# Rows of x: written in token order and gathered per expert tile, instead of scattered into expert order

## The chip, the core and the metric

The kernel runs on one core of a Trainium2 chip. The metric is the device time of one execution in microseconds (us). PE is TensorE, DVE is VectorE, ACT is ScalarE, POOL is GpSimd, SP is the sync engine, which here only starts DMA transfers.

## What is computed

Attention without a softmax, then a mixture of 8 experts in which each token goes to one expert, then a gated linear layer:

```python
kv = np.einsum('bhsd,bhse->bhde', k, v)                 # batch 8, heads 8, seq 576, dim 64
out = np.einsum('bhsd,bhde->bhse', q, kv)
x = out / sqrt(mean(out * out, axis=-1) + 1e-6) * g_norm  # as [4608, 512]
logits = x @ w_gate + modality_bias[modality_id]         # 8 experts
e_idx = argmax(logits); gate = softmax(logits)[e_idx]
for e in range(8):                                       # 512 -> 1024 -> 512
    out[e_idx == e] = gate * (relu(x[e_idx == e] @ w1[e]) @ w2[e])
out = (sigmoid(out @ wg_gate) * (out @ wg_val)) @ w_out  # 512 -> 1536 -> 512
```

Products with large weights are made in three passes of float32r parts (high times high, high times low, low times high), so "high" and "low" copies are made of weights and activations.

## The kernel before, in words

There are three stages on the same engines, each engine with its own instruction stream.

**Attention.** 36 steps ("slots" run from 0 to 42, with fixed lags) treat 72 chunks of 128 half tokens, two chunks a slot: partitions 0 to 63 hold the first four heads of 64 tokens and partitions 64 to 127 the other four heads of the same tokens. In a slot PE makes the output of one pair of chunks (L1006), transposes the q of a later one (L1029), ACT squares the output, copies the transposed q (L566) and prepares the next q (L584), DVE sums the squares (L828), takes the reciprocal (L808), writes the normalised rows to `xb` (L815) and the scaled products with the gate weights to `lgh` (L822). At the start of a batch of 4.5 slots PE makes k times v with 144 small matmuls (L1042). SP loads k, v and q of a batch and raw expert weights, all on its one queue.

**Routing.** The 72 chunks form nine groups of 4, 8, 12, 12, 12, 8, 8, 4, 4 (`GROUPS`). When a group's last chunk is done, PE folds the two halves into logits (L1060, 5 slots later), DVE finds the expert and counts (`route_part`, slot 6), PE ranks over the partitions (L1066, L1067), and DVE computes each token's row in its expert's region of the DRAM tensor `x_rows` (`place_part`, slot 7, last instruction L793). POOL then issues one indirect DMA per chunk (L462), 128 rows of 1088 bytes each: half of x, and behind it the token's number. `xb` holds 36 chunks, so a group's rows wait there for their places. After the last group, the token counts are turned into tables (L837 to L860), and eight DMAs of zeros fill each expert's last, partly filled tile (`zero_pads`, L385, four from SP and four from ACT), each behind a register load. Then the first tile of x can be read.

**Experts.** 40 tiles of 128 rows. POOL reads a tile with four plain DMAs (`load_x`, L482), reads its token numbers (`load_tok`, L486), gathers their gates with an indirect DMA (`gather_gate`, L490) and scatters the finished rows (`scatter`, L496). DVE turns x (`x_turned`), makes low parts, splits the next expert's weights (L740, L746), and multiplies with the gate (`y_of`). PE multiplies (L1090 up, L1112 down). The loop over the full tiles is a hardware loop with two tiles in its body; the first tile and the last ones are written out.

**Gated layer.** Nine blocks of 512 tokens (L1136 and L1147), at the end of which POOL scatters each 128 rows by `out_tok`.

Waits are on semaphores. SP's and POOL's streams are in program order: what stands behind a wait waits too.

## Time and profile before

| what | value |
|---|---|
| median of 3 runs | 1635.85 us (1634.67 to 1637.78) |
| profiled execution, its time | 1633.38 us |
| profiled execution, its span | 1631.4 us |
| mean granted clock of PE | 0.948 |
| busy share of the span: PE, DVE, ACT, POOL | 92%, 36%, 23%, 19% |

The span is from the first to the last instruction; the 2.0 us between it and the execution's time lie around it. A busy share is a mean over three stages that are limited in different ways, so the stages have to be read one by one. In the rows, "idle before <-issue" is time in which an engine waited for nothing that the profile shows.

### The profile page before, as it was taken

How to read it: one execution, taken by the hardware profiler on the slowest of the kernel's cores; microseconds unless marked ns; L12 is line 12 of the kernel's file. 1: busy time of each engine (PE TensorE's matmuls, PEld its weight loads, DVE VectorE, ACT ScalarE, POOL GpSimd, SP SyncE). 2: the span in 40 equal slices, each digit the busy share in tenths (PEclk: the TensorE clock that was granted, in tenths of full speed). 3: DMA queues.
4: the chain of work that ended last, by engine and by line, in shares of the span. 5: the costliest groups of instructions: out<-in, count | busy, mean ns of one | idle time of the engine just before them, and what ended most of it. 6: DMA issues, size and time to landing. Idle time of an engine off the chain costs nothing.

```text
span 1631.4 us, 25528 instructions
## 1 busy us (share of the span) xinstructions
PE 1505.4 (92%) x8836; PEld 1234.1 (76%) x8837; DVE 584.1 (36%) x1095; ACT 380.4 (23%) x698; POOL 311.8 (19%) x402
## 2 busy tenths in 40 slices
PE   5765549999999999989999999999999999999997
PEld 4544438888888888868888888888888888888885
DVE  4444366457645665334411212122121211212111
ACT  4443312222221212223311211112121111212111
POOL 0223354444444444310000000000000000000000
PEclk8676559999999999999999999999999999999998
DMA  9555234245423443315300201002010100100000
GB/s 330 202 210 187 72 124 146 75 116 150 127 84 97 138 122 96 102 57 127 80 27 1 52 1 27 27 2 51 0 27 27 27 26 0 27 26 1 26 0 26
DMA packets 78612, 124.07 MB, mean 76 GB/s; under 512 B 17342, under 2 KB 41918, under 8 KB 78528
## 3 DMA queue, kind: packets, MB, share of 16 engines
q1 hardware_dynamic: 56576, 80.85, 16.8%
q0 software_dynamic: 17216, 39.75, 7.6%
q10 hardware_dynamic: 4736, 2.26, 0.6%
q8 instruction: 63, 1.03, 0.3%
q14 instruction: 21, 0.17, 0.0%
HBM read 91.38 MB, written 32.52 MB: 76 GB/s over the span
## 4 chain that ended last, share of the span: by engine, by line
PE 88%; issue 6%; DVE 2%; ACT 1%; DMA 1%; another core or an unknown queue 1%; SPq 0%; POOLq 0%; POOL 0%; ACTq 0%; DVEq 0%
PE ps L1136 37%; PE ps L1147 18%; PE ps L1112 13%; PE ps L1090 13%; PE ps L1042 2%; PE ps L1099 2%; PE ps L1029 1%; PE ps L1006 1%; DMA vt<-in_v 1%; ACT qp L584 0%; DVE ew L746 0%; DMA x_rows<-zero 0%; DVE xb L815 0%; DVE ssum L828 0%
## 5 line engine op out<-in xcount | busy, mean ns | idle before, releaser
L1136 PE MATMUL ps<-yhi,gv 128*128 128x512 f32 x1728 | 557.0, 393 | 6.5 <-DVE wo L967 5.8
L1136 PEld LDWEIGHTS ps<-yhi,gv 128*128 128x128 f32 x1728 | 325.3, 188 | 79.2 <-DVE wo L967 6.2
L1136 PE MATMUL ps<-ylo,gv 128*128 128x512 f32 x864 | 339.4, 393 | 0.0
L1147 PE MATMUL ps<-wo,shi 128*128 128x512 f32 x864 | 266.8, 390 | 1.4 <-DVE slo L984 1.4
L982 DVE TENSOR_TENSOR s<-ps,sig 128x512 f32<-128x512 f32 x108 | 74.7, 691 | 472.0 <-ACT sig L666 467.3
L1090 PE MATMUL ps<-ew,xhi 128*128 x640 | 202.4, 397 | 4.5 <-DVE xlo L891 3.2
L529 POOL DMA_INDIRECT out<-ot,out_tok x36 | 34.5, 960 | 870.4 <-ACT ot L681 864.6
L1112 PE MATMUL ps<-ew,hhi 128*128 x640 | 197.1, 389 | 1.3 <-DVE hlo L908 1.3
L1136 PEld LDWEIGHTS ps<-ylo,gv 128*128 128x128 f32 x864 | 162.6, 188 | 37.8 <-issue 1.1
L1147 PEld LDWEIGHTS ps<-wo,shi 128*128 128x128 f32 x864 | 162.1, 188 | 36.9 <-DVE slo L984 1.9
L666 ACT ACTIVATE sig<-ps 128x512 f32<-128x512 f32 x108 | 64.5, 597 | 494.8 <-PE ps L1136 486.1
L1147 PE MATMUL ps<-wo,slo 128*128 128x512 f32 x432 | 168.3, 390 | 0.0
L984 DVE TENSOR_TENSOR slo<-s,shi 128x512 fp32r<-128x512 f32 x108 | 74.8, 692 | 214.5 <-ACT shi L669 214.5
L1112 PEld LDWEIGHTS ps<-ew,hhi 128*128 128x128 f32 x640 | 120.1, 188 | 26.4 <-issue 1.5
L1090 PEld LDWEIGHTS ps<-ew,xhi 128*128 128x128 f32 x640 | 118.0, 189 | 29.0 <-issue 6.1
L1090 PE MATMUL ps<-ew,xlo 128*128 x320 | 125.7, 393 | 0.0
L1112 PE MATMUL ps<-ew,hlo 128*128 x320 | 124.8, 390 | 0.0
L669 ACT CAST shi<-s 128x512 fp32r<-128x512 f32 x108 | 67.1, 622 | 226.7 <-PE ps L1147 225.9
L482 POOL DMA_DIRECT2D xg<-x_rows x160 | 90.8, 568 | 150.0 <-issue 145.1
L462 POOL DMA_INDIRECT x_rows<-xb,r_idx x72 | 69.5, 965 | 156.9 <-DVE r_idx L793 137.1
L1147 PEld LDWEIGHTS ps<-wo,slo 128*128 128x128 f32 x432 | 81.1, 188 | 17.1
L746 DVE SCALAR_TENSOR_TENSOR ew<-raw,g_tab,ew 128x1024 f32 (+1 forms) x64 | 82.2, 1284 | 8.4 <-DVE ew L740 4.3
(159 smaller groups left out, 1214.8 us busy)
## 6 DMA issues: line engine op xcount, KB each, us to landing
raw<-in_moe_w SPq DMA_DIRECT2D x64, 512.0 KB
xg<-x_rows POOLq DMA_DIRECT2D x160, 64.0 KB
kt<-in_k SPq DMA_DIRECT2D x8, 1152.0 KB, 5.7
vt<-in_v SPq DMA_DIRECT2D x8, 1152.0 KB, 9.6
qt<-in_q SPq DMA_DIRECT2D x8, 1152.0 KB, 5.4
yin<-y_rows SPq DMA_DIRECT2D x32, 256.0 KB, 5.3
graw<-in_moe_w_gate SPq DMA_DIRECT2D x6, 512.0 KB, 3.8
graw<-in_moe_w_val SPq DMA_DIRECT2D x6, 512.0 KB, 4.8
```

What stands on the lines that cost most here:

```text
L462: nc.gpsimd.indirect_dma_start(out=x_rows, out_offset=bass.IndirectOffsetOnAxis(ap=r_idx[:, c:c + 1], axis=0), in_=xb[:, c % RING, :], in_ ...
L482: nc.gpsimd.dma_start(xg[32 * g:32 * g + 32, t.p], src.rearrange("(t j) x -> j t x", j=32)).then_inc(x_in[t.p], 16)
L529: nc.gpsimd.indirect_dma_start(out=out, out_offset=bass.IndirectOffsetOnAxis(ap=out_tok[:, 4 * b + m:4 * b + m + 1], axis=0), in_=ot[:, m] ...
L666: nc.scalar.activation(sig[:], ps[:, 2 * (f % 2), :], ACT.Sigmoid).then_inc(sig_made, 1)
L669: nc.scalar.copy(shi[:], s32[:]).then_inc(shi_made, 1)
L746: made = nc.vector.scalar_tensor_tensor(out=lo_part, in0=raw[:, u, cols], scalar=g_tab[:, bass.ds(qn % 4, 1)], in1=hi_part.bitcast(F32), o ...
L982: nc.vector.tensor_tensor(s32[:], ps[:, 2 * (f % 2) + 1, :], sig[:], ALU.mult).then_inc(s_made, 1)
L984: nc.vector.tensor_tensor(slo[:], s32[:], shi[:].bitcast(F32), ALU.subtract).then_inc(slo_made, 1)
L1090: last = mm(ps[:, 1 + f, :], x[:, t.p, rows], weights(e, c, part, cols), start=first, stop=end)
L1112: last = mm(ps[:, 5, :], x[:, rows], weights(e, DC + c // 2, part, cols), start=first, stop=end)
L1136: last = mm(ps[:, 2 * (f % 2) + part, :], gv[f // 2][:, w, part, d, cols], x[c % 2][:, d, :], start=first, stop=end)
L1147: last = mm(ps[:, 4 + m, :], s[:, rows], wo[f // 2][:, w, f % 2], start=(f == 0 and s is shi and w == 0), stop=(f == GC - 1 and s is slo))
```

## The change

The rows of x no longer go to expert order in DRAM. SP stores each pair of chunks as it is finished, in token order and without the token number (36 stores, 40 DMAs, of 256 KB a pair; a row of x is split into four rows of 512 bytes); `xb` shrinks to 8 chunks. `xb` is written after `lgh` instead of before it, and PE's next output waits for `xb`. There are six groups of 12 chunks.

To know which token stands where in expert order, a token list is built: for each pair of chunks POOL makes three one-hot tiles (`hots`: 128, 288 and 288 columns, bf16) from the place's remainder and quotient by 128, with the token's number split in two parts as factor; PE adds their products up over the group (12 matmuls, 9 slots after the group's end), DVE adds the group to `order` (10 slots). For the last group POOL and DVE make three pairs each. Then four matmuls with selection matrices and four DVE instructions turn `order` into row addresses (`row_of`), and each tile's column is copied to `row_now` (`aim`) and `seat_now` (`seat_aim`) by DVE with a column number from a register.

In the expert stage POOL issues four indirect gathers of 512-byte rows for a tile of x; the read of token numbers is gone. The zero pads are gone. `compact_rows` is moved behind the first two `x_turned`. At the eighth step of the first gated block DVE turns list numbers into token numbers (`tokens`, five instructions). SP's loads of attention are written out slot by slot among the stores.

```diff
-    CAP = N + 128
-    XW = D // 2 + 16
+    CAP = (N + 127) // 128 * 128
...
+    HALF = D // 2
...
-    RING = 36
+    RING = 8
...
-    GROUPS = [(0, 4), (4, 8), (12, 12), (24, 12), (36, 12), (48, 8), (56, 8), (64, 4), (68, 4)]
+    GROUPS = [(c, 12) for c in range(0, T, 12)]
...
-    LAG_RANK, LAG_PLACE = LAG_LG + 1, LAG_LG + 2
-    SLOTS = S + LAG_PLACE
+    LAG_RANK, LAG_PLACE, LAG_ORDER, LAG_KEEP = LAG_LG + 1, LAG_LG + 2, LAG_LG + 4, LAG_LG + 5
+    SLOTS = S + LAG_KEEP
+    LAST = len(GROUPS) - 1
...
+    x_v = x_rows.rearrange("(b p j g) x -> b p j (g x)", b=BATCH, j=J, g=2)
...
-    x_row = keep("x_row", [1, NT + 1], I32)
-    pad_row = keep("pad_row", [1, E], I32)
-    zero = keep("zero", [128, 2 * XW], F32)
+    x_col = keep("x_col", [1, NT + 1], I32)
+    seat_of = keep("seat_of", [128, QN], U32)
+    row_of = keep("row_of", [128, 4, QN], U32)
...
-    xb = att("xb", [128, RING, XW], F32)
+    xb = att("xb", [128, RING, HALF], F32)
...
-        def zero_pads(engine, e):
-            row = engine.value_load(pad_row[0:1, e:e + 1], min_val=e * CAP, max_val=e * CAP + N)
-            engine.dma_start(x_v[bass.ds(row, 128)].rearrange("w n x -> w (n x)"), zero[:]).then_inc(pads_out[0 if e == 0 else 1], 16)
+        def hots(engine, g, k):
+            pair = PG * g + k
+            engine.tensor_scalar(hot_r[:, k, :], across[:, 0:128], spot_r[:, g % 2, k:k + 1], None, ALU.is_equal)
+            engine.tensor_scalar(hot_q[:, k, 0, :], across[:], spot_q[:, g % 2, k:k + 1], seat_low[:, pair:pair + 1], ALU.is_equal, ALU.mult)
+            return engine.tensor_scalar(hot_q[:, k, 1, :], across[:], spot_q[:, g % 2, k:k + 1], seat_high[:, pair:pair + 1], ALU.is_equal, ALU.mult)
         @block.sync
...
+            def load_kv(b):
...
                 load(vt, v_v, b, v_in)
-                if b >= 2:
-                    sp.wait_ge(qp_made, (J * (b - 1) + 1) // 2)
-                load(qt, q_v, b, q_in)
-                if 1 <= b <= EARLY:
-                    load_raw(sp, 0, b - 1)
+            def store(o):
+                sp.wait_ge(x_normed, 2 * o + 2)
+                at = 2 * o % RING
+                b, j = 2 * o // J, 2 * o % J
+                if spans_two(o):
+                    sp.dma_start(x_v[b, :, j], xb[:, at, :]).then_inc(x_out[o % (RING // 2)], 16)
+                    sp.dma_start(x_v[b + 1, :, 0], xb[:, at + 1, :]).then_inc(x_out[o % (RING // 2)], 16)
+                else:
+                    sp.dma_start(x_v[b, :, j:j + 2], xb[:, at:at + 2, :]).then_inc(x_out[o % (RING // 2)], 16)
+            load_kv(0)
+            load(qt, q_v, 0, q_in)
+            load_kv(1)
+            load(qt, q_v, 1, q_in)
+            load_raw(sp, 0, 0)
+            load_kv(2)
+            for s in range(S + LAG_NORM + 1):
...
+                    if s == (J * (b - 1) + 1) // 2:
+                        sp.wait_ge(qp_made, s)
+                        load(qt, q_v, b, q_in)
+                        if b <= EARLY:
+                            load_raw(sp, 0, b - 1)
+                        if b + 1 < BATCH:
+                            load_kv(b + 1)
+                o = s - LAG_NORM - 1
+                if o >= 0:
+                    store(o)
             for unit in range(EARLY, UNITS):
                 load_raw(sp, 0, unit)
-            sp.wait_ge(pads_made, 1)
...
-            for e in range(E // 2):
-                zero_pads(sp, e)
             sp.wait_ge(gates_made, 1)
-            sp.dma_start(gates.rearrange("(b p j) a -> p b (j a)", p=R, j=J), r_val[0:R].rearrange("p (b j) -> p b j", b=BATCH)).then_inc(gates_out, 16)
+            sp.dma_start(gates_v, r_val[:].rearrange("p (b j) -> p b j", b=BATCH)).then_inc(gates_out, 16)
             sp.wait_ge(gates_out, 16)
...
+                pool.wait_ge(iota_made, 9 + n)
+                nc.gpsimd.iota(seat_i[R * n:R * n + R], [[2 * SEQ, BATCH], [1, J]], base=0, channel_multiplier=J).then_inc(iota_made, 1)
+            pool.wait_ge(iota_made, 11)
+            pool.wait_ge(seat_made, 1)
+            for g in range(len(GROUPS)):
+                wait(pool, pe_order, g)
+                pool.wait_ge(spot_made, g + 1)
+                for k in range(PG // 2 if g == LAST else PG):
+                    hots(nc.gpsimd, g, k).then_inc(hot_made, 1)
+            for n in range(RING // 2):
+                pool.wait_ge(x_out[n], stored(S - RING // 2 + n))
             def when(sem_, count):
                 wait(pool, sem_, count)
                 pool.sem_inc(turn, 1)
-            def row_of(t):
-                return pool.value_load(x_row[0:1, bass.ds(t.n, 1)], min_val=0, max_val=E * CAP - 128)
-            def load_x(t, row=None):
+            def load_x(t):
                 when(xt_made, t.n - 1)
-                row = row_of(t) if row is None else row
-                for g in range(4):
-                    src = x_v[bass.ds(row, 128), g // 2, 128 * (g % 2):128 * (g % 2) + 128]
-                    nc.gpsimd.dma_start(xg[32 * g:32 * g + 32, t.p], src.rearrange("(t j) x -> j t x", j=32)).then_inc(x_in[t.p], 16)
-            def load_tok(t):
-                row = row_of(t)
-                nc.gpsimd.dma_start(tok_now[:, t.p:t.p + 1], tok_v[bass.ds(row, 128)], allow_slow_non_contiguous=True).then_inc(t_in[t.p], 16)
+                when(aim_made, t.n + 1)
...
+                        in_offset=bass.IndirectOffsetOnAxis(ap=row_now[:, t.p, m:m + 1], axis=0)).then_inc(x_in[t.p], 16)
             def gather_gate(t):
-                when(t_in[t.p], 16 * (t.half + 1))
+                when(seat_aimed, t.n + 1)
                 nc.gpsimd.indirect_dma_start(
                     out=gate_now[:, t.p:t.p + 1], out_offset=None, in_=gates,
-                    in_offset=bass.IndirectOffsetOnAxis(ap=tok_now[:, t.p:t.p + 1], axis=0)).then_inc(gate_in[t.p], 16)
+                    in_offset=bass.IndirectOffsetOnAxis(ap=seat_now[:, t.p:t.p + 1], axis=0)).then_inc(gate_in[t.p], 16)
...
-            load_x(Tile(0, 0), 0)
+            load_x(Tile(0, 0))
             pool.sem_inc(x_asked, 1)
             pool.wait_ge(tables_made, 1)
-            pool.wait_ge(pads_out[1], 16 * (E - 1))
...
                     use(Tile(i, c - 2), scatter)
-                use(Tile(i, c), load_tok)
-                if c > 0:
-                    use(Tile(i, c - 1), gather_gate)
+                use(Tile(i, c), gather_gate)
             for n in range(2):
...
-            pool.wait_ge(tok_in, 16)
+            pool.wait_ge(tok_step, 5)
...
-            act.wait_ge(pads_made, 1)
-            for e in range(E // 2, E):
-                zero_pads(act, e)
...
+                wait(dve, pe_order, g - 1)
+                for n in range(2):
+                    part = slice(R * n, R * n + R)
+                    then(nc.vector.tensor_copy(spot_i[part], r_p[part, 0:m].rearrange("p (k two) -> p k two", two=2)[:, :, n]))
+                then(nc.vector.tensor_scalar(spot_qi[:], spot_i[:], 7, None, ALU.logical_shift_right))
+                nc.vector.tensor_copy(spot_q[:, g % 2], spot_qi[:])
+                nc.vector.scalar_tensor_tensor(out=spot_r[:, g % 2], in0=spot_qi[:], scalar=-128.0, in1=spot_i[:],
+                                               op0=ALU.mult, op1=ALU.add).then_inc(spot_made, 1)
+                if g == LAST:
+                    dve.wait_ge(spot_made, g + 1)
+                    wait(dve, pe_order, g)
+                    for k in range(PG // 2, PG):
+                        hots(nc.vector, g, k).then_inc(last_hot_made, 1)
             steps[0] = 0
             def then(ins):
                 chain(route_step, ins)
+            def keep_order(g):
+                dve.wait_ge(pe_order, g + 1)
+                if g == 0:
+                    kept = nc.vector.tensor_copy(order[:], ps[:, 3, ORDER])
+                else:
+                    dve.wait_ge(order_kept, g)
+                    kept = nc.vector.tensor_tensor(order[:], order[:], ps[:, 3, ORDER], ALU.add)
+                kept.then_inc(order_kept, 1)
...
+                if s - LAG_KEEP in ENDS:
...
-                        old = group_of(2 * o - RING)
-                        dve.wait_ge(x_out[old], 16 * GROUPS[old][1])
                     dve.wait_ge(rstd_made, o + 1)
...
-                            outs(o)[:, :, jj, 0:DH].rearrange("p h (g i) -> p h g i", g=2),
-                            scale[:, :, jj].unsqueeze(2).unsqueeze(3).to_broadcast([128, PAIRS, 2, 32]), ALU.mult).then_inc(x_normed, 1)
                     g = group_of(2 * o)
                     wait(dve, pe_lg, g - 1)
                     at = 2 * o - GROUPS[g][0]
                     nc.vector.tensor_tensor(lgh[:, g % 2, :, at:at + 2, :], outs(o)[:, :, :, DH:KX],
                                             scale.unsqueeze(3).to_broadcast([128, PAIRS, 2, E]), ALU.mult).then_inc(lgh_made, 1)
+                    if o >= RING // 2:
+                        dve.wait_ge(x_out[o % (RING // 2)], stored(o - RING // 2))
+                    for jj in range(2):
+                        nc.vector.tensor_tensor(
+                            xb[:, 2 * o % RING + jj, :].rearrange("p (g h i) -> p h g i", g=2, h=PAIRS),
+                            outs(o)[:, :, jj, 0:DH].rearrange("p h (g i) -> p h g i", g=2),
+                            scale[:, :, jj].unsqueeze(2).unsqueeze(3).to_broadcast([128, PAIRS, 2, 32]), ALU.mult).then_inc(x_normed, 1)
                 o = s - LAG_OUT
...
-            dve.wait_ge(idx_made, len(GROUPS))
+            dve.wait_ge(order_kept, len(GROUPS))
+            nc.vector.tensor_copy(seat_of[:], order[:])
+            for m in range(4):
+                dve.wait_ge(pe_pick, m + 1)
+                last = nc.vector.tensor_scalar(row_of[:, m, :], ps[:, 4 + m, 0:QN], shift[:], None, ALU.add)
+            last.then_inc(rows_made, 1)
+            dve.wait_ge(rows_made, 1)
+            nc.vector.tensor_copy(row_now[:, 0, :], row_of[:, :, 0]).then_inc(aim_made, 1)
+            nc.vector.tensor_copy(seat_now[:, 0:1], seat_of[:, 0:1]).then_inc(seat_aimed, 1)
             nc.vector.memset(r_unit[:], 1.0)
...
+            def column(t):
+                return dve.value_load(x_col[0:1, bass.ds(t.n, 1)], min_val=0, max_val=QN - 1)
+            def aim(t):
+                nc.vector.tensor_copy(row_now[:, t.p, :], row_of[:, :, bass.ds(column(t), 1)].rearrange("p m a -> p (m a)")).then_inc(aim_made, 1)
+            def seat_aim(t):
+                wait(dve, y_made, t.n - 1)
+                nc.vector.tensor_copy(seat_now[:, t.p:t.p + 1], seat_of[:, bass.ds(column(t), 1)]).then_inc(seat_aimed, 1)
             def xlo_of(t):
                 dve.wait_ge(xhi_made, t.n + 1)
...
                 wait(dve, y_out[t.p], 16 * t.half)
-                dve.wait_ge(t_in[t.p], 16 * (t.half + 1))
+                dve.wait_ge(seat_aimed, t.n + 1)
                 nc.vector.tensor_copy(to_now[:, t.p:t.p + 1], to_i[:, bass.ds(t.n, 1)])
-                nc.vector.tensor_copy(y[:, t.p, D:D + 1].bitcast(I32), tok_now[:, t.p:t.p + 1].bitcast(I32))
+                nc.vector.tensor_copy(y[:, t.p, D:D + 1].bitcast(I32), seat_now[:, t.p:t.p + 1].bitcast(I32))
                 dve.wait_ge(pe_y, t.n + 1)
...
+                use(Tile(i, c + 1), seat_aim)
                 use(Tile(i, c + 2), x_turned)
+                use(Tile(i, c + 4), aim)
             def y_turned(i, c):
...
                     nc.vector.tensor_tensor(ylo[c % 2][:, :, cols], yt[c % 2][:, :, cols],
                                             yhi[c % 2][:, :, cols].bitcast(F32), ALU.subtract).then_inc(ylo_made, 1)
+            aim(Tile(0, 1))
             nc.vector.memset(y[:, :, D:YW], 0.0)
-            compact_rows()
             gate_values()
             use = Use(dve)
             x_turned(Tile(0, 0))
+            aim(Tile(0, 2))
             xlo_of(Tile(0, 0))
             x_turned(Tile(0, 1))
+            aim(Tile(0, 3))
+            compact_rows()
...
+            def tokens():
+                dve.wait_ge(tok_in, 16)
+                steps[0] = 0
+                chain(tok_step, nc.vector.tensor_scalar(tok_b[:], out_tok[:], 7, None, ALU.logical_shift_right))
+                chain(tok_step, nc.vector.tensor_scalar(tok_b[:], tok_b[:], 57.0, None, ALU.mult))
+                chain(tok_step, nc.vector.tensor_scalar(tok_b[:], tok_b[:], 9, None, ALU.logical_shift_right))
+                chain(tok_step, nc.vector.tensor_scalar(tok_b[:], tok_b[:], float(SEQ), None, ALU.mult))
+                chain(tok_step, nc.vector.tensor_tensor(out_tok[:], out_tok[:], tok_b[:], ALU.subtract))
...
-                    wait(pe, lgh_made, o - 1)
+                    wait(pe, x_normed, 2 * (o - 1))
...
-                    wait(pe, lb_made, g)
-                    wait(pe, off_made, len([e for e in ENDS if e <= ENDS[g] - 2]))
+                    wait(pe, off_made, g)
+                    wait(pe, order_kept, g - 1 if ENDS[g] - ENDS[g - 1] < LAG_KEEP - LAG_LG else g)
...
+                if s - LAG_ORDER in ENDS:
+                    g = ENDS.index(s - LAG_ORDER)
+                    for k in range(PG):
+                        if g == LAST and k >= PG // 2:
+                            pe.wait_ge(last_hot_made, k - PG // 2 + 1)
+                        else:
+                            pe.wait_ge(hot_made, PG * g + k + 1)
+                        for part in range(2):
+                            last = mm(ps[:, 3, ORDER], hot_r[:, k, :], hot_q[:, k, part, :], start=(k == 0 and part == 0), stop=(k == PG - 1 and part == 1))
+                    last.then_inc(pe_order, 1)
+            pe.wait_ge(x_normed, T)
+            pe.wait_ge(order_kept, len(GROUPS))
+            for m in range(4):
+                mm(ps[:, 4 + m, 0:QN], pick[:, m, :], order[:], start=True, stop=True).then_inc(pe_pick, 1)
             pe.wait_ge(acc_made, len(GROUPS))
             mm(ps[:, 3, TOTAL], ones[:], acc[0:R], start=True, stop=True).then_inc(pe_counts, 1)
```

## Rows read from the trace of the kernel before

**Rows 1.** Windows by stage: busy time (matmuls), granted clock, DMA share, GB/s.

```profile
core 0: us, PE busy (x) PEld busy (x) DVE busy (x) ACT busy (x) POOL busy (x), PEclk, DMA share, GB/s
0.00:203.00 203.00, 121.35 (x2608) 97.83 (x2609) 88.15 (x292) 81.01 (x184) 55.48 (x70) 0.71 0.57 201
...
219.80:241.00 21.20, 5.07 (x6) 1.85 (x6) 11.71 (x42) 2.58 (x3) 10.98 (x15) 0.58 0.52 172
...
250.30:715.00 464.70, 462.83 (x2192) 385.15 (x2193) 254.02 (x390) 109.30 (x201) 195.26 (x263) 1.00 0.38 110
715.00:1631.00 916.00, 898.00 (x3906) 733.94 (x3904) 211.57 (x305) 182.70 (x302) 35.63 (x38) 0.99 0.11 29
```

**Rows 2.** Waits of PE from 250 to 700 us: total, times, longest.

```profile
PE ps L1090 <- DVE ew L746: 0.7, 1, 0.7
```

**Rows 3.** Waits of PE from 59.5 to 203 us.

```profile
PE ps L1042 <- issue: 24.2, 35, 2.2
PE ps L1006 <- issue: 18.3, 26, 1.7
...
PE ps L1029 <- issue: 3.9, 7, 1.0
```

**Rows 4.** Windows: three bursts of twelve scatters, and two stretches between.

```profile
89.50:108.00 18.50, 7.45 (x122) 4.89 (x116) 1.35 (x4) 0.79 (x3) 11.51 (x12) 0.59 0.40 148
108.00:125.50 17.50, 13.64 (x377) 11.31 (x376) 13.38 (x44) 13.43 (x33) 0.12 (x1) 0.92 0.66 228
125.50:143.50 18.00, 7.99 (x104) 5.40 (x104) 4.22 (x14) 3.42 (x8) 11.40 (x12) 0.57 0.62 233
143.50:158.50 15.00, 10.72 (x290) 9.17 (x286) 10.47 (x34) 9.57 (x23) 0.00 (x0) 0.83 0.37 116
158.50:179.00 20.50, 11.16 (x203) 8.22 (x207) 3.26 (x9) 2.31 (x7) 11.52 (x12) 0.51 0.23 83
```

**Rows 5.** Timeline in one burst: start, us, engine and line, idle before.

```profile
89.51 0.95 POOL L462 DMA_INDIRECT x_rows<-xb,r_idx  x1 [19.96 <-DVE r_idx L793]
...
93.81 0.49 PE L1042 MATMUL ps<-vt,kt 64*64 64x64 f32 x5 [0.63 <-issue]
...
95.24 0.50 PE L1042 MATMUL ps<-vt,kt 64*64 64x64 f32 x4 [0.95 <-issue]
```

**Rows 6.** Groups of instructions on POOL in the first 41 us.

```profile
L447 POOL IOTA ident_i<- 128x128 int32 x1 | 0.2, 229 | 0.4 <-POOLq L1178 0.4
...
L450 POOL IOTA pri_i<- 128x8 int32 x1 | 0.1, 124 | 0.0
```

**Rows 7.** Timeline of PE: one group's logits, eight matmuls of 96 columns.

```profile
81.10 1.03 PE L1060 MATMUL ps<-lgh,fold 128*128 128x96 f32 x8
```

**Rows 8.** DMA issues of the page: KB of one, us from issue to landing.

```profile
vt<-in_v SPq DMA_DIRECT2D x8, 1152.0 KB, 9.6
```

**Rows 9.** Groups of the expert stage: busy us, mean ns, idle before.

```profile
L482 POOL DMA_DIRECT2D xg<-x_rows x145 | 82.0, 566 | 139.1 <-issue 134.5
...
L490 POOL DMA_INDIRECT gate_now<-gates,tok_now x40 | 49.5, 1236 | 15.1 <-issue 14.4 <-DVE xt L886 0.7
...
L896 DVE COPY to_now<-to_i 128x1 uint32 (+1 forms) x39 | 6.0, 153 | 44.7 <-issue 44.7
```

**Rows 10.** The tile of gates in the expert stage: landing of its gathers.

```profile
DMA to landing us min/median/max: 2.2/2.7/6.9
```

**Rows 11.** Timeline from the last logits' input to the second tile.

```profile
209.34 0.21 DVE L822 TENSOR_TENSOR lgh<-ps,rstd 128x64 f32<-128x64 f32 x1
...
219.69 0.23 DVE L793 TENSOR_SCALAR r_idx<-r_p,half 128x4 uint32<-128x4 f32 x1
...
222.94 10.06 SPq L385 DMA_DIRECT2D x_rows<-zero  x4
...
232.74 5.07 PE L1123 MATMUL ps<-zero,ident 128*128 128x512 f32 x6 [13.01 <-POOLq L502]
...
250.27 0.72 PE L1090 MATMUL ps<-ew,xhi 128*128 x2 [0.71 <-DVE ew L746]
```

115 lines of the change are left out of this document (73 added, 42 removed).

## The prediction

> **What bounds the kernel now.** I read the windows by stage first, because a busy share over the whole span mixes three stages. In the expert stage PE is busy 462.8 of 464.7 us, in the gated layer 898.0 of 916 [rows 1]. Between 250 and 700 us PE waited for another engine 0.7 us in all [rows 2]. So after 250 us nothing in the change can win; it can only lose. What can be won lies before: 203 us of attention in which PE is busy 121 us at a granted clock of 0.71, and the 41 us from the last logits' input (209.3) to the second tile (250.3) [rows 1, 11].
>
> Second I read PE's waits in attention. Nearly all are put down to "issue", no engine: 24.2 + 18.3 + 3.9 = 46.4 us [rows 3]. The windows show when. In the three bursts of twelve scatters PE ran 122 + 104 + 203 = 429 matmuls in 57.0 us, 7.5 per us, and POOL was busy with its scatters; in the two stretches between, 667 in 32.5 us, 20.5 per us [rows 4]. The DMA share is not the cause by itself: 0.40, 0.62 and 0.23 in the bursts, 0.66 and 0.37 between. The timeline shows the form: the first scatter issues at 89.51, and from 93.8 us on PE gets four or five matmuls, then nothing for nearly 1 us, within matmuls that have no wait of their own [rows 5]. The granted clock is 0.51 to 0.59 in the bursts (near the 1.2 GHz level), 0.92 and 0.83 between (mostly at 2.4) [rows 4]. My reading: while POOL's scatters run, PE gets its instructions slowly. At 20.5 per us the 429 matmuls would take 20.9 us, so 36 scatters cost 36.1 us, 1.0 us each.
>
> **The change, part by part.** Sums are made against the profiled execution, 1633.4 us (span 1631.4 and 2.0 around it); the median is 2.5 above it.
>
> *72 scatters in attention go.* By PE's own issue waits this gives back 46.4 us; by 1.0 us per scatter and the 56 scatters of the first six groups (4 + 8 + 12 + 12 + 12 + 8, all issued before 203) 56; if a third of the issue waits have other causes, 31. I take 46.
>
> *36 stores on SP's queue come.* Each is 256 KB in runs of 2 KB, 9.4 MB in all, like the scatters' 10 MB. First cost: a store stands behind the q load, one raw load and the k and v of a batch, 3968 KB. k and v, 2304 KB, land in 9.6 us [rows 8], so that block takes up to 16.5 us. `xb` now holds four slots; a slot was 209.3 / 40 = 5.2 us [rows 11] and would be 4.3, so 17 us of cover. DVE waits 0 to 3 us at each of six blocks, and behind DVE's wait stand the sum of squares, ACT's root, PE's next output: +5 (0 to 18). Second cost: stores may slow the instruction supply as scatters do. No row shows a plain write under attention; nearest are plain loads, beside which PE runs at full rate at a DMA share of 0.66 [rows 4]. I take +3; the other end, 1.0 us per store, is a rival.
>
> *The token list.* PE gets twelve matmuls per group; eight of 96 columns in fp32 take 1.03 us [rows 7], 0.13 each, so 1.6 per group, up to double at the low clock; five groups are inside attention, where PE has holes anyway: +5 (0 to 16). POOL's tiles have 128 + 288 + 288 = 704 columns a pair. POOL shows only iotas: 229 ns for 128 columns, 124 for 8, so 0.12 us fixed and 0.9 ns a column [rows 6]; a pair is at least 1.0 us, and I take 1.3, 7.8 us a group. PE needs them two slots after DVE has the places, 8.6 us. The cover just holds; I take 0.6 a group, +3 (0 to 40: behind PE's wait stand its own outputs, so a late list is paid in full). The Trainium skill, GPSIMD Reference, section 3, "Performance versus the Vector engine", speaks against this part: elementwise work belongs on VectorE, and a two-input add of 2048 columns takes 4497 ns on GpSimd. By that figure an estimate for a pair is 1.5 us and the fixed parts, 1.9, and a group 11.5, so PE would wait 3 us five times and the time be 12 us above my sum. No row here decides.
>
> *Six groups for nine.* Three passes of the logits' matmuls fewer, 1.0 us each [rows 7]; DVE's fewer passes pay for its four new small instructions and `keep_order`: -3 (-10 to +3).
>
> *The tail.* Before: 40.7 us from the end of `lgh` to the second tile, of which 10.4 are routing (209.55 to 219.92), and most of the rest the last scatters, the pads (SP's four end at 233.0) and the loads [rows 11]. After: 10.4; four small instructions, 1; nine one-hot instructions on DVE at 0.2 to 0.4, or three pairs on POOL, 4; last products and `keep_order`, 1.3; four matmuls of 288 columns (three of 512 took 5.07 us, so 0.95 each) and addresses, 4.5: 21.2. Then the longer of four gathers (3 x 1.5 and 2.7 to land, 7.2 [rows 9, 10]) and DVE's tables and gate values, about 8 of the 11.7 us that it was busy in this stretch [rows 1]; turning and splitting x, 2; the first tile 7 and a gap, 2: 40. The pads' 10 us are thus spent on building the list. 0 (-6 to +8). What is late next is DVE: with the pads gone, the tables end last, not a transfer.
>
> *Expert stage.* POOL's four plain loads (0.57 us) and the token read become four gathers (1.24 and 0.3 between) [rows 9]: with the gate and the y scatter 6 x 1.54 = 9.2 us of a tile's 11.8 (464.7 us for 39.4 tiles). It fits, and a tile is asked for two tiles ahead, so the cover is a whole tile; without it, each tile costs what POOL exceeds 11.8. DVE gets two register loads and two copies a tile; a copy is 0.15 and the idle before one with a register load 1.1 [rows 9], so +1.3 or so a tile, beside a DVE busy 254 of 465 us. It was late once, by 0.7 us; in tiles with two splits it may be late again: +2 (0 to 10).
>
> *Gated layer.* `tokens` is five small instructions of DVE in the first block, 1.2 us, under PE's products (898.0 of 916 busy): 0. POOL's scatters wait for them, but the first has data only at the block's end.
>
> Sum: -46 + 5 + 3 + 5 + 3 - 3 + 0 + 2 = -31, so 1602.4 for the profiled execution and about 1604 to 1605 for the median; I say 1604.
>
> **Rivals.**
> *A, 0.60, the forecast*: 1578 to 1620. The low end is 56 given back and half the costs.
> *B, 0.19: the stores hold PE as well.* For: both are writes to DRAM on the same DMA engines. Against: SP's queue needs nothing of POOL. Half the gain back: 1622 to 1632, centre 1626. The Trainium skill, DMA: Bandwidth & Descriptors, section "Queues, rings and completion order", says that a DMA engine takes turns between its queues packet by packet; by my reading that makes no difference between a scatter and a store.
> *C, 0.07: POOL's lists are late.* It turns the sign when a pair costs over (31 / 5 + 0.6 + 8.6) / 6 = 2.6 us; at 3.5 the groups wait 12 us each, 5 x 12 = 62: 1663.
> *D, 0.05: the gathers stretch the tiles.* Against: POOL's 9.2 of 11.8. In the last written-out tiles, instructions have to be fetched beside the gathers, six indirect DMAs each. It decides from 0.8 us a tile (40 tiles); at 1.3, 1604 + 50 = 1654.
> *E, 0.06: the holes aren't the scatters'.* Then nothing is won and the costs stay: 1635.9 + 15 = 1651. Against it: 7.5 to 20.5 matmuls per us, three times over [rows 4]. The Trainium skill, Runtime: NRT & Kernel Launch, section "Instruction fetch mechanics", says that fetching is hidden behind the issue of instructions; by it the holes would not be supply at all, and this case would hold. The trace speaks against it: holes of nearly 1 us inside matmuls without waits [rows 5].
> The remaining 0.03 is spread on both sides.
>
> **Numbers.** 0.2% is about what measurements of this kernel can tell. Faster: A, B and 0.02, 0.81. Within 0.2% (1632.6 to 1639.1): the edges of B, D and E, 0.05. Slower: the rest of C, D and E, 0.14. The range 1576 to 1634 holds A and B, and with them 8 in 10.
>
> **What would show it.** The windows of attention at 18 to 20 matmuls per us throughout, PE's issue waits under 15 us, last `lgh` near 177 us; DVE waiting for `x_out` under 2 us a batch; PE waiting for POOL's one-hot tiles about 0.6 us a group; second tile 41 us behind the last `lgh`; tiles at 11.8 us. Wrong if PE's holes stay and move to the stores (B), if PE's order matmuls wait over 8 us (C), or if PE is idle between 250 and 700 us (D).

## The result and the profile after

The changed kernel takes 1695.5 us (median of four runs, 1691.6 to 1705.0), the kernel before 1635.3 beside it (1634.5 to 1637.8): ratio 1.0374, 95% interval 1.0326 to 1.0423. I had forecast 1604 and a range up to 1634. The change costs 60 us where I expected it to give 31. The first eight kernels below were each executed once, the later ones mostly two times or more; stage lengths come from the one profiled execution of each.

The first view is again the windows by stage, of the profiled execution (1692.2 us), cut at the last `lgh`, the second tile and the first gated matmul:

```profile
core 0: us, PE busy (x) PEld busy (x) DVE busy (x) ACT busy (x) POOL busy (x), PEclk, DMA share, GB/s
0.00:218.70 218.70, 119.55 (x2712) 93.09 (x2713) 95.79 (x320) 85.05 (x189) 99.83 (x105) 0.73 0.52 188
218.70:265.00 46.30, 25.05 (x72) 15.39 (x72) 24.61 (x84) 4.00 (x7) 23.09 (x22) 0.60 0.18 47
265.00:774.30 509.30, 479.21 (x2208) 392.57 (x2208) 271.57 (x478) 112.67 (x204) 230.54 (x227) 0.98 0.34 101
774.30:1690.00 915.70, 902.75 (x3888) 729.75 (x3888) 206.18 (x300) 180.15 (x299) 35.05 (x36) 0.99 0.11 29
```

Before, the same four cuts lie at 213.2, 250.3, 724.8 and 1631.4. The 209.3 on which my prediction counted the tail [rows 11] was the last `lgh` but one; the last follows at 213.2. So the 59.0 us of longer span are:

| stage | before | after | difference |
|---|---|---|---|
| attention, to the last `lgh` | 213.2 | 218.7 | +5.5 |
| tail, to the second tile | 37.1 | 46.3 | +9.2 |
| expert stage, to the first gated matmul | 474.5 | 509.3 | +34.8 |
| gated layer, to the end | 906.7 | 916.1 | +9.4 |

The second view is PE's waits from 59.5 us to the last `lgh`, which answers to [rows 3]:

```profile
PE ps L1197 <- POOL hot_q L424: 48.4, 22, 3.0
PE ps L1126 <- issue: 12.8, 11, 2.5
PE ps L1186 <- DVE r_cnt L840: 5.3, 4, 1.4
```

The waits named issue, all lines together, went from 46.4 to 14.2 us, and in their place stand 48.4 us for POOL's one-hot lists. The groups of POOL's instructions in attention give the price of one, and the timeline shows PE taking a pair each time POOL has finished one (PE's next product starts 3.2 us behind the last, with 2.5 to 2.8 us idle ahead of it):

```profile
L424 POOL TENSOR_SCALAR hot_q<-across,spot_q,seat_high 128x288 bf16<-128x288 f32 x30 | 40.9, 1363 | 0.0
L423 POOL TENSOR_SCALAR hot_q<-across,spot_q,seat_low 128x288 bf16<-128x288 f32 x30 | 40.0, 1334 | 0.0
L422 POOL TENSOR_SCALAR hot_r<-across,spot_r 128x128 bf16<-128x128 f32 x30 | 18.1, 604 | 116.5 <-DVE spot_r L862 116.5
```

```profile
109.21 0.66 PE L1197 MATMUL ps<-hot_q,hot_r 128*128 128x288 bf16 x2 [2.79 <-POOL hot_q L424]
112.42 0.66 PE L1197 MATMUL ps<-hot_q,hot_r 128*128 128x288 bf16 x2 [2.54 <-POOL hot_q L424]
```

A pair takes POOL 0.60 + 1.33 + 1.36 = 3.3 us. The pairs start 3.2 us apart, so a group of six takes 19.3 us, and two slots lie between the indices and the products.

The third view is DVE's waits in the expert stage, 265 to 760 us:

```profile
DVE to_now L999 <- issue: 48.9, 37, 6.2
...
DVE hlo L1011 <- issue: 25.8, 17, 2.8
DVE hlo L1011 <- ACT hhi L689: 22.7, 16, 2.9
...
DVE seat_now L990 <- issue: 19.9, 12, 1.9
```

`hlo` is the low half of the hidden activations that PE's down product waits for. Seventeen times DVE stood still ahead of it, for 1.5 us on average, with no engine named. What that is, the experiments had to tell.

PE's own waits in the stage (270 to 735 us) name something else, and the timeline of all engines shows what is behind the longest of them:

```profile
PE ps L1234 <- ACT h L684: 11.3, 8, 2.0
PE ps L1225 <- issue: 7.3, 12, 0.9
PE ps L1247 <- issue: 3.9, 6, 1.0
```

```profile
302.12 0.70 DVE L978 STREAM_TRANSPOSE xt<-xg 128x512 f32<-128x512 f32 x1
...
302.85 0.62 ACT L677 CAST xhi<-xt 128x512 fp32r<-128x512 f32 x1 [6.89 <-DVE xt L978]
...
303.37 1.08 ACT L684 ACTIVATE h<-ps 128x512 f32<-128x512 f32 x2
...
304.02 1.14 PE L1234 MATMUL ps<-ident,h 128*128 128x128 f32 x8 [1.98 <-ACT h L684]
```

DVE comes late to turning the next tile's x (`xt`). ACT's copy `xhi` waits for it, in program order ACT's `h` stands behind that copy, and PE's transposes (L1234) wait for `h`. So a DVE that runs late reaches PE by way of ACT.

### The profile page after: what moved, and what is told of

The parts are those of the page before. It is cut to its first block, busy times and chain, and to the rows that moved or that the text cites. A ratio compares the mean times of both kernels' runs of the same rounds, so it can differ in the third digit from the quotient of the medians.

```text
span 1690.4 us, 25450 instructions
## 1 busy us (share of the span) xinstructions
PE 1526.6 (90%) x8880; PEld 1230.8 (73%) x8881; DVE 598.1 (35%) x1179; ACT 381.9 (23%) x698; POOL 388.5 (23%) x390
## 4 chain that ended last, share of the span: by engine, by line
PE 75%; POOL 7%; DVE 5%; issue 5%; DVEq 3%; another core or an unknown queue 2%; ACT 1%; DMA 1%; POOLq 0%; ACTq 0%; SPq 0%
PE ps L1271 35%; PE ps L1282 18%; PE ps L1247 8%; PE ps L1225 8%; POOL hot_q L424 3%; POOL hot_q L423 3%; PE ps L1234 2%; DVE ew L804 1%; POOL hot_r L422 1%; DVEq L1019 1%; PE ps L1149 1%; PE ps L1162 1%; DVEq L983 1%; PE ps L1126 1%
## 5 line engine op out<-in xcount | busy, mean ns | idle before, releaser
L1282 PE MATMUL ps<-wo,shi 128*128 128x512 f32 x864 | 271.4, 395 | 1.4 <-DVE slo L1104 1.4
L1225 PE MATMUL ps<-ew,xhi 128*128 x640 | 205.9, 404 | 11.3 <-issue 7.3
L540 POOL DMA_INDIRECT xg<-x_rows,row_now x160 | 160.1, 1001 | 59.7 <-issue 48.9
L677 ACT CAST xhi<-xt 128x512 fp32r<-128x512 f32 x40 | 24.8, 620 | 248.5 <-DVE xt L978 248.5
## 6 DMA issues: line engine op xcount, KB each, us to landing
vt<-in_v SPq DMA_DIRECT2D x8, 1152.0 KB, 11.3
```

The costliest lines, as they stand in the source:

```text
L540: nc.gpsimd.indirect_dma_start(out=xg[:, t.p, m, :], out_offset=None, in_=x_rows, in_offset=bass.IndirectOffsetOnAxis(ap=row_now[:, t.p, m ...
L1225: last = mm(ps[:, 1 + f, :], x[:, t.p, rows], weights(e, c, part, cols), start=first, stop=end)
L1282: last = mm(ps[:, 4 + m, :], s[:, rows], wo[f // 2][:, w, f % 2], start=(f == 0 and s is shi and w == 0), stop=(f == GC - 1 and s is slo))
```

## The experiments

Stages are given as last `lgh` / tail / expert stage / gated layer, in us. The chips turned out to matter, so each run's kernel before is named with it. In the expectations, B and C are the prediction's rivals; D-gather and D-DVE are the two culprits that the expert stage could have, the gathers on POOL or the register loads and copies on DVE.

**The lists on DVE.**

```
+            return 0 if g == LAST else 0
...
-                for k in range(PG // 2 if g == LAST else PG):
+                for k in range(on_pool(g)):
...
-                if g == LAST:
+                if on_pool(g) < PG:
...
-                    for k in range(PG // 2, PG):
+                    for k in range(on_pool(g), PG):
```

> All six pairs of one-hot lists of each group are made by DVE in place of POOL; nothing else differs from the changed kernel. Theory C (POOL's lists are late: 59.7 us of PE's waits for hot_q and 64.7 us of DVE's waits for the order matmuls behind them in the changed kernel): the four slots of 13.5 to 16.6 us fall to 3 to 9 us (a pair costs DVE 1.0 us, six of them 6 us), the last lgh ends at 175 to 195 us in place of 218.7, and the time is 1650 to 1675 us. Rival B (the stores of x hold the engines whatever makes the lists): the last lgh stays at 210 to 225 us and the time at 1685 to 1700 us.

1661.1 us (before 1632.6): 193.4 / 41.6 / 508.0 / 916.3. Attention loses 25.3 us of its length though DVE took over 33 pairs; one of DVE's costs 0.28 + 0.42 + 0.42 = 1.1 us, a third of POOL's:

```profile
L427 DVE TENSOR_SCALAR hot_q<-across,spot_q,seat_low 128x288 bf16<-128x288 f32 x30 | 12.7, 424 | 0.0
L428 DVE TENSOR_SCALAR hot_q<-across,spot_q,seat_high 128x288 bf16<-128x288 f32 x30 | 12.7, 423 | 0.0
L426 DVE TENSOR_SCALAR hot_r<-across,spot_r 128x128 bf16<-128x128 f32 x30 | 8.4, 280 | 0.2
```

Rival C holds; B falls as the main cause. PE's waits named issue are now 48.6 us, 13 times, up to 7.6 us. They are not the short holes of before: one of 4.9 us ends at 101.65, just behind DVE's `xb` (100.80 to 101.54), which DVE makes only after six pairs of lists.

**Plain loads of x in the expert stage.**

```
-                    nc.gpsimd.indirect_dma_start(
-                        out=xg[:, t.p, m, :], out_offset=None, in_=x_rows,
-                        in_offset=bass.IndirectOffsetOnAxis(ap=row_now[:, t.p, m:m + 1], axis=0)).then_inc(x_in[t.p], 16)
+                    nc.gpsimd.dma_start(xg[:, t.p, m, :], x_rows[128 * m:128 * m + 128]).then_inc(x_in[t.p], 16)
```

> The four gathers of x of an expert tile are four plain transfers of fixed rows (so every tile multiplies the same 512 rows of half-heads and the result of the tiles is left out of the computation); the index copies on DVE stay. Attention as in the changed kernel. Theory D-gather (the gathers hold the engines' instructions or delay the tiles): the stretch from the second tile to the first gated matmul falls from 509.3 us to 470 to 490. Rival D-DVE (the two register loads and copies that DVE makes for a tile lengthen the tiles in which DVE also splits weights): it stays at 500 to 512 us.

1657.6 us (before 1632.6): 218.6 / 46.2 / 474.6 / 916.4. The expert stage has its old length back, with DVE's register loads in place. (This kernel leaves out the reading of the right rows, so only its times mean anything.)

**The register loads and copies on POOL.** POOL reads `x_col` and writes `row_now` and `seat_now` itself, just ahead of its gathers; `aim` and `seat_aim` leave DVE.

> The register loads and the copies of row_now and seat_now are made by POOL just before its gathers, in place of DVE; the gathers stay. Rival D-DVE: the stretch from the second tile to the first gated matmul falls from 509.3 us to 474 to 490 and the time by 20 to 35 us. Theory D-gather: it stays at 500 to 515 us, and if POOL's own copies come late it grows.

1659.6 us (before 1632.6): 218.8 / 46.5 / 476.7 / 915.8. The stage is short again, with the gathers in place. So on this chip the loss went when either of the two was gone (476.7 and 474.6 against 508.0 in the lists-on-DVE kernel beside them). The two theories, each of which named one culprit, were both half right.

**The register loads in the kernel before.**

```
+            def aim(t):
+                nc.vector.tensor_copy(row_spare[:, t.p, :], zero[:, 0:32].rearrange("p (m e) -> p m e", m=4)[:, :, bass.ds(column(t), 1)].rearrange("p m a -> p (m a)"))
+
+            def seat_aim(t):
+                nc.vector.tensor_copy(seat_spare[:, t.p:t.p + 1], zero[:, bass.ds(column(t), 1)])
```

> The kernel before, with two register loads and two small copies added on DVE for each expert tile, at the places where the changed kernel has them; what they copy is used by nothing. D-DVE: the stretch from the second tile to the first gated matmul grows from 474.5 us to 490 to 510. D-gather: it stays within 5 us of 474.5. Attention does not change (the last lgh at 209.5 us).

1625.2 us (before 1632.6): 214.5 / 36.3 / 475.0 / 897.8. Beside plain loads the same two register loads cost nothing. (The 209.5 of the expectation is the last `lgh` but one of the first profile; its last is at 213.2.) The gated layer is 8.9 us shorter, though only two small tiles ahead of its buffers were added (128 bytes).

**The weights moved in SBUF.**

```
+    keep.at += 2368
     ew_base = keep.at
```

> The changed kernel with 2368 bytes left free ahead of the weights in SBUF, so that ew, gv0 and wo0 start at the same offset modulo 8192 bytes as in the kernel before; nothing else. In the gated layer the changed kernel takes 916.1 us against 906.7 before, and its output matmuls start 0.2325 to 0.2333 us apart against 0.2267 to 0.2283. Placement theory: they are back at 0.2267 to 0.2283 us and the layer takes 906 to 909 us. Rival: the layer stays at 914 to 918 us, and the cause lies elsewhere (the places of shi and slo, or the instruction stream).

1652.0 us: 219.0 / 46.3 / 477.8 / 907.1; the kernel before took 1582.4 on this chip. The placement theory holds for the gated layer: back from 916 to 907 us. The groups of the output products, of the changed kernel first, show 395 and 390 ns for one (in a block of twelve near 1150 us the starts lie 0.2336 us apart in the first, 0.2273 to 0.2282 in the second):

```profile
L1282 PE MATMUL ps<-wo,shi 128*128 128x512 f32 x764 | 239.9, 395 | 0.0
```

```profile
L1283 PE MATMUL ps<-wo,shi 128*128 128x512 f32 x776 | 239.4, 390 | 0.0
```

But the expert stage, which this edit does not touch, is short as well, and the kernel before is 50 us faster than on the first chips.

**The order products later.**

```
-    LAG_RANK, LAG_PLACE, LAG_ORDER, LAG_KEEP = LAG_LG + 1, LAG_LG + 2, LAG_LG + 4, LAG_LG + 5
+    LAG_RANK, LAG_PLACE, LAG_ORDER, LAG_KEEP = LAG_LG + 1, LAG_LG + 2, LAG_LG + 9, LAG_LG + 10
...
+                    pe.wait_ge(off_made, min(g + 2, len(GROUPS)))
+                    wait(pe, order_kept, g)
```

> The order matmuls of a group are issued nine slots behind its logits in place of four, so that POOL's 19.3 us of lists lie beside seven slots of PE's other work in place of two. Theory C: PE's waits for hot_q fall from 59.7 us to under 15, no slot is over 8 us, the last lgh ends at 170 to 190 us; the last two groups' lists then come right behind each other, so that the tail grows from 46.3 us to 47 to 65. Time 1650 to 1680 us. Rival B: the last lgh stays at 210 to 225 us.

1625.8 us (before 1582.4): 175.6 / 56.2 / 475.8 / 916.2. With seven slots of cover PE no longer waits for POOL's lists in attention at all, and the last `lgh` ends 43 us sooner. The tail grows by 9.9 us, since POOL makes most of the last two groups' lists there (PE's 16.2 us of waits for them, a little over the 15 I had named, all lie behind 181 us). The time lies under the range I gave, which I had counted with an expert stage of 509 us.

**Later, and shared.** One pair of each group and five of the last group's six on DVE; the function below gives the pairs that POOL makes:

```
+            return 1 if g == LAST else 5
```

> As the later order matmuls, and DVE makes one pair of lists of each group and five of the last group's six (POOL the rest). Theory C: the last lgh ends at 170 to 190 us, the lists of the last group are ready some 6 us behind their indices in place of 10, so the second tile starts 40 to 46 us behind the last lgh. Time 1635 to 1670 us. Rival B: the last lgh stays at 210 to 225 us.

1617.2 us (before 1582.4): 178.6 / 45.0 / 475.2 / 916.5. The tail is back at 45.0. The time lies under what I expected, by the 34 us of the expert stage that this chip does not lose.

**A ring of sixteen.** `RING = 16` for 8, in the changed kernel.

> The changed kernel with sixteen blocks in the ring of normed rows that the stores read, in place of eight. Rival B (stores that are late hold DVE and behind it PE): DVE's 8.1 us of waits for the stores go and the last lgh ends 5 to 15 us sooner than 218.7. Theory C: the waits go over to POOL's lists; the last lgh stays within 3 us of 218.7, and the time within 5 us of the changed kernel's profiled 1692.

1658.2 us (before 1582.4): 215.0 / 46.8 / 478.7 / 915.8. DVE's 8.1 us of waits for the stores are gone, but attention gains only 3.7 us, between the 3 of theory C and the 5 of rival B: as long as the lists are late, the ring is hardly what is waited for. The time misses "within 5 us of 1692", since the expert stage is short here.

**The changed kernel, the kernel before and the loads on POOL, once more, and a first combination.** The combination has the later and shared lists, the loads on POOL, and `seat_now`, `row_now` (128 bytes) and the weights (2496 bytes) moved.

> The changed kernel itself, once more. Its stretch from the second tile to the first gated matmul was 509.3 us in the profile, yet 478 to 479 us in two kernels that leave that stretch alone (the moved weights, the ring of sixteen), on a chip where the kernel before took 1582 us in place of 1633. Theory D-DVE with gathers (DVE's register loads wait for instructions beside the gathers, on some chips): on a chip where the kernel before takes 1630 to 1638 us, the stretch is 505 to 512 us and the time 1688 to 1700. Rival (the stretch is long or short by chance, in any execution of it): single times of this kernel on one chip lie 25 us or more apart.

> The kernel before itself, once more, for its stages on this chip: last lgh at 209.5 us (of the transposed kind), the stretch from the second tile to the first gated matmul 474.5 us, the gated layer 906.7 us where the chip is as the first; where the kernel takes some 1582 us, PE's waits named issue in attention (46.4 us in the first profile) fall under 10 us.

> The register loads and copies made by POOL, once more, beside the changed kernel on one chip. D-DVE with gathers: 25 to 40 us under the changed kernel where that has the long stretch, and under 5 us where it has the short one. Rival (chance): the two kernels' times overlap.

> Order matmuls nine slots behind the logits, one pair of lists of each group and five of the last group's on DVE, the register loads and copies on POOL, seat_now and row_now moved by 128 bytes and the weights by 2496 bytes (so that the tiles of the gated layer lie modulo 8192 as in the kernel before with aims, whose gated layer took 897.8 us). By the stages of the runs so far: last lgh 178.6, tail 45, expert stage 475, gated layer 898 to 907, together 1597 to 1606 us and 2 around it: 1598 to 1612, under the kernel before (1633) by 1.3 to 2.2%. If the removed scatters had given nothing (Rival E), the attention would be at 200 us or more and the time over 1625.

All on one chip: changed kernel 1660.8 us (218.4 / 46.4 / 476.6 / 916.9), kernel before 1580.3 (160.6 / 34.4 / 474.6 / 908.0), loads on POOL 1659.8 (218.8 / 46.6 / 476.7 / 915.9), combined 1599.1 (178.3 / 43.5 / 477.2 / 897.5). Here the change costs 5.0% (1.0504, interval 1.0480 to 1.0527), and the loads on DVE or POOL make no difference. Nearly all that the kernel before gains here is attention (213.2 to 160.6); its expert stage and gated layer are as on the first chips, within 1.3 us:

```profile
669.61 0.79 PE L1136 MATMUL ps<-yhi,gv 128*128 128x512 f32 x1 [5.80 <-DVE wo L967]
```

The kernel before has fewer holes here: a window over twelve scatters (to be held against the bursts of [rows 4]) and PE's issue waits from 59.5 us on, 16.1 us in all where I had expected under 10 and the first profile has 46.4:

```profile
102.40:117.40 15.00, 9.92 (x288) 8.07 (x289) 9.38 (x25) 9.63 (x21) 11.54 (x12) 0.77 1.02 362
```

```profile
PE ps L1006 <- issue: 9.0, 13, 1.5
...
PE ps L1042 <- issue: 3.4, 3, 1.5
PE ps L1051 <- issue: 2.1, 1, 2.1
```

288 matmuls in 15.0 us are 19.2 per us, against 7.5 in the bursts of the first profile, at a larger DMA share (1.02). The code, the scatters (0.96 us each) and their bytes are the same. So I speak of two kinds of chip: on one, PE loses much time beside POOL's indirect transfers, on the other little. Each chip was used for one set of runs only, so a lasting property of the chip can't be told here from one of the time of measuring.

The changed kernel on this chip shows what the first kind costs the expert stage. Its stage as a window, and three of DVE's waits (265 to 740 us):

```profile
264.80:741.36 476.56, 466.21 (x2208) 388.00 (x2208) 272.54 (x478) 111.72 (x203) 224.56 (x227) 1.00 0.37 108
```

```profile
DVE y L1003 <- PE ps L1247: 65.0, 37, 4.8
...
DVE seat_now L990 <- issue: 20.5, 12, 1.9
...
DVE hlo L1011 <- issue: 0.4, 1, 0.4
```

With the same 2208 matmuls PE is busy 466.2 us here and 479.2 in the first profile, and idle 10.4 against 30.1. The waits ahead of `seat_now` are as long as there (20.5, 19.9) and so cost nothing by themselves; those ahead of `hlo` are gone (25.8 to 0.4).

**The same on a chip of the first kind.**

> The changed kernel once more. Chips so far fall in two kinds by the kernel before: 1632 to 1638 us (last lgh at 213.2 in its profile) or 1577 to 1586 us (last lgh at 160.6). If this is a chip of the first kind: theory (engines wait for their instructions beside POOL's indirect transfers on such chips): attention as ever (last lgh 218 to 219), the stretch from the second tile to the first gated matmul 500 to 512 us, time 1685 to 1705. Of the second kind: that stretch 476 to 479 us, time 1657 to 1663.

> Register loads and copies of the expert tiles on POOL, a third time. First kind of chip: the stretch from the second tile to the first gated matmul 475 to 480 us and the time 25 to 40 us under the changed kernel on this chip. Second kind: within 5 us of it. If the stretch is long here too, the short one of the first time was chance.

> The combined kernel on another chip. By its stages (attention has no scatters, so no holes by them): 1595 to 1605 us on both kinds of chip, so 1.7 to 2.4% faster than the kernel before where that takes 1633, and 0.9 to 1.4% slower where that takes 1580.

> The combined kernel with sixteen blocks in the ring of normed rows in place of eight. In the combined kernel DVE waits 15.8 us in attention for the stores of x (four times, the longest 6.3) and PE 39.5 us behind it by the name issue. Rival B (once POOL's lists are hidden, the stores through a ring of eight are the next wait): the last lgh ends 8 to 20 us sooner than 178.3, and the time is 8 to 20 us under the combined kernel's. Else it stays within 3 us.

The kernel before took 1636.5 us. Changed kernel 1692.2 (218.9 / 48.5 / 504.5 / 916.2), loads on POOL 1660.3 (219.5 / 46.6 / 477.3 / 917.1), combined 1598.6 (178.5 / 43.6 / 477.9 / 897.7), combined with a ring of sixteen 1588.6 (167.7 / 43.7 / 478.6 / 896.8). All four as expected. DVE's waits in the expert stage, of the changed kernel and of the loads on POOL:

```profile
DVE hlo L1011 <- issue: 25.1, 19, 2.9
```

```profile
DVE hlo L1012 <- ACT hhi L701: 8.9, 28, 0.4
...
DVE hlo L1012 <- issue: 2.5, 8, 0.4
```

The waits with no engine named ahead of `hlo` are 25.1 us with the loads on DVE and 2.5 without; PE's waits for ACT's `h` are 8.2 and 2.8 us (270 to 735 us). Combined against before is 0.9775 (0.9754 to 0.9795); with the larger ring 0.9711 (0.9698 to 0.9724). The ring's 10.8 us appear only now, when the lists are in time.

**The last two, on a further chip of the first kind.**

> The combined kernel with the ring of sixteen, on another chip. By its stages on the chip of the first kind (last lgh 167.7, tail 43.7, expert stage 478.6, gated layer 896.8) it has no stage that depends on the kind: 1585 to 1592 us on both. So 2.7 to 3.1% faster than the kernel before where that takes 1633 to 1638, and 0.2 to 0.9% slower where that takes 1577 to 1586.

> The same with the register loads and copies back on DVE. Theory (on chips of the first kind DVE's instructions for the expert tiles wait beside the gathers): first kind, the stretch from the second tile to the first gated matmul is 500 to 512 us and the time 22 to 35 us over the other kernel of this call; second kind, 475 to 480 and within 5 us. Rival (the loss in that stretch belongs to the other parts of the changed kernel, such as the list's lateness): no difference on either kind.

The kernel before took 1631.9 us. Combined with the ring 1588.4 (168.7 / 43.5 / 477.4 / 897.0), ratio 0.9736 (0.9714 to 0.9758); with the loads back on DVE 1617.9 (166.2 / 45.0 / 506.8 / 897.6). 29.4 us of the 29.5 lie in the expert stage, and DVE's waits have the same line again:

```profile
DVE hlo L1021 <- issue: 25.4, 20, 2.4
```

## Why the prediction was wrong, step by step

Two steps failed, and either would have been enough: the price of the list (some 45 us) and the expert stage (some 33). Tail and gated layer added 9 us each.

*The scatters' holes.* My 46 us (31 to 56) hold, on chips of the first kind: PE's issue waits fell by 32, and the same kernel before reaches its last `lgh` 52.6 us sooner on a chip where the scatters hold PE little (213.2 against 160.6). With the lists out of the way the last `lgh` comes at 175.6 to 178.6 us, where I had forecast 177. Rival E is out. That PE's stream is slow beside the scatters is what the traces show; that it is instruction supply stays my reading. The Trainium skill, Runtime: NRT & Kernel Launch, section "Instruction fetch mechanics", has fetching hidden behind the issue of instructions; the second kind of chip agrees with that (19.2 matmuls per us beside scatters), the first kind (7.5) does not, if these holes are fetching. I never asked whether it would be so on every chip.

*The list.* This is the first and larger of the steps that failed: "POOL shows only iotas: ... a pair is at least 1.0 us, and I take 1.3". A pair takes 3.3 us. I worked from an instruction that reads nothing (0.9 ns a column); one that reads fp32 and writes bf16 takes 4.6 to 4.7 ns a column (604 ns at 128 columns with one operation, 1334 at 288 with two). The Trainium skill, GPSIMD Engine Reference, section 3, "Performance versus the Vector engine", from whose figure I had worked out an estimate of 1.9, spoke in the right direction; the measured 3.3 decides. My own rival C had the mechanism, the place and a turning point of 2.6 us; I gave it 0.07. With 3.3 in its formula the wait is 6 x 3.3 - 9.2 = 10.6 us a group, 53 for five: measured 48.4 on PE. The later products take 43 us off attention and so carry the proof (175.6 against 218.4 to 218.9 in every run of the changed kernel). The mistake was to take the value next to the lower bound in a step where the upper bound stood at 40 us and the cover was used up to 0.8 us. PE's own part was priced rightly, 1.6 us a group: with its lists ready, the lists-on-DVE kernel makes twelve products in 1.63 us.

*The stores.* For the wait that a ring of eight brings I had +5 (0 to 18); a ring of sixteen takes away 3.7 us while the lists are late, 10.8 when they are not. My +3 for stores that hold PE (rival B) was not measured by itself. It is unlikely to be much: in the combined kernel with the larger ring the last `lgh` ends at 167.7 us, against 160.6 for the kernel before on the chip with few holes, and these 7.1 us hold the list's products and the copies behind them as well.

*The tail.* 0 (-6 to +8) came to +9.2. POOL's three pairs take from 226.75 to 237.0 us (I had counted 4), at up to 1.65 us an instruction while DVE makes its own three, which are done by 229.6; DVE then stands for 9.6 us, to 239.2:

```profile
229.15 0.42 DVE L424 TENSOR_SCALAR hot_q<-across,spot_q,seat_high 128x288 bf16<-128x288 f32 x1
...
235.70 1.33 POOL L424 TENSOR_SCALAR hot_q<-across,spot_q,seat_high 128x288 bf16<-128x288 f32 x1
237.07 1.57 PEld L1197 LDWEIGHTS ps<-hot_q,hot_r 128*128 128x128 bf16 x8 [3.07 <-POOL hot_q L424]
237.08 2.10 PE L1197 MATMUL ps<-hot_q,hot_r 128*128 128x288 bf16 x8 [2.54 <-POOL hot_q L424]
239.22 0.45 DVE L882 TENSOR_TENSOR order<-order,ps 128x288 f32<-128x288 f32 x1 [9.64 <-PE ps L1197]
```

`row_now` is written 26 us behind the last `lgh` where I had counted 21, and the whole is 46.3 where I had 40: mostly the list's price once more. The other 2.9 us of the 9.2 are a slip of mine: the tail before is 37.1 and not 40.7, since I counted it from the last `lgh` but one. With one pair on POOL the tail is 43.5 to 45.0.

*The expert stage.* This is the second step that failed: "It fits, and a tile is asked for two tiles ahead", with DVE's new work priced by itself. +2 (0 to 10) came to +34.8 in the profile, 504.5 to 508.0 in three further cases on chips of the first kind (one of them the combined kernel with the loads on DVE, 506.8), and only 475.2 to 478.7 on chips of the second kind. I had costed both parts rightly by themselves: gathers with the loads on POOL take 476.7 and 477.3 us, 2 to 3 over the 474.5 before, and register loads without gathers 475.0. Together, on chips of the first kind, they cost 27 to 31 us (508.0, 504.5 and 506.8 against 476.7, 477.3 and 477.4 with the loads on POOL). Rival D had the place, but its price hung on POOL's pace, and POOL was not the limit: it is busy 230.5 of 509.3 us. I had even written that indirect transfers slow an engine's instructions, for PE in attention, and for the last written-out tiles in rival D, and did not apply it to DVE in the loop into which the change moves most of the 160 gathers. The 48.9 us ahead of `to_now` were there before (44.7, [rows 9]), and so are waits ahead of `seat_now` where nothing is lost; new are those ahead of `hlo`. They use up DVE's slack: ahead of `y`, where it otherwise waits for PE's down product in 37 tiles, it waits in only 23 (under all names, 265 to 760 us). Where DVE has no slack left it is late with `xt`, and PE waits behind ACT's `h` (11.3 us in place of 1.6, 270 to 735 us). That chain explains the waits that name ACT. For the rest of the 33 us between the two profiles, PE's waits that name nobody and the 13.0 us of longer busy time at a granted clock of 0.98 in place of 1.00, I have no cause shown.

*The gated layer.* 0 came to +9.4. The step "under PE's products" was right about `tokens`, but the products themselves became slower, since the change moved the buffers in SBUF. Moving the weights gives back 9.0. The length goes with the places and not with the chip: the kernel before has 906.7 and 908.0 us on chips of either kind, the kernels with the changed kernel's places 915.8 to 917.1, the kernel before with aims and the combined ones 896.8 to 897.8. By what rule the place matters stays open.

*The sum*, on the first kind: -52.6 for the holes, +58.1 for list and stores in attention, +9.2, +34.8, +9.4: +58.9 against +59.0 in the span. The first two are differences to the 160.6 us of the other chip, so they add up by themselves; of the 58.1, some 51 went by experiment (218.9 to 167.7 with later, shared lists and the larger ring).

What stays open: what sets the two kinds of chip apart (of five chips three were of the first, two of the second; the first comparison was of the first kind too by its time), and whether a chip keeps its kind, and by what path POOL's indirect transfers slow PE and DVE. On the first kind the holes come with the transfers and go with them; that the engines' instructions are late is the reading that fits waits with no engine named, and no run here isolates it. Whether the combined kernel, at 1588 us, is a little slower than the kernel before on the second kind (1580) was not timed with the ring of sixteen, since both chips it ran on were of the first kind; with eight it was, 1.0116 (1.0098 to 1.0135).

## What to carry to other kernels

When work moves to an engine for which the trace has no instruction of its kind, the price is open on the upper side; if the cover beside it is nearly used up, take the upper bound as seriously as the lower and ask at which price the sign turns. A mechanism found in one stage (here: engines are slow beside POOL's indirect transfers) has to be carried into every stage into which the change moves its cause, and set against the engine with the least slack there. And where a late step is fixed, look for the next wait behind it: the lists hid the ring, and only both together brought attention from 219 to 168 us.

## What the hardware showed that I had not expected

The kernel before differs by over 3% between chips (medians 1580 and 1582 against 1632 to 1637 us), with its times on one chip within 0.6% of each other; nearly all of it is attention, with 7.5 against 19.2 matmuls per us beside indirect scatters. A POOL tensor_scalar of 288 columns from fp32 to bf16 takes 1334 to 1363 ns, the same on DVE 424. Register loads on DVE cost nothing beside plain loads (475.0 us a stage), nor beside gathers on the second kind of chip (476.6), and 27 to 31 us beside gathers on the first. The fp32r matmuls of 512 columns in the output products start 0.2336, 0.2273 to 0.2282 or 0.2264 us apart, by the place of their tiles in SBUF (blocks of twelve near 1150 us of the changed kernel, of the kernel before and the moved weights, and of the combined kernel). The gated layer of 3888 matmuls of 512 columns took 916, 907 or 897 us, and moving the weights by 2368 bytes alone was worth 9.0 of it.
